# A spare PSUM bank for every second up step behind the attention, and x split in halves

## The reference

```python
scores = scale * np.matmul(q, k.transpose(0, 1, 3, 2))
kth = np.partition(scores, -top_k, axis=-1)[..., -top_k:-top_k + 1]      # top_k = 32
scores = np.where(scores >= kth, scores, -1000000000.0)
attn = softmax(scores)                                                   # over the last axis
x = (attn @ v), heads side by side                                       # 2304 tokens x 512
h = x @ w_in                                                             # 512 x 2048
g = np.where(h >= 1, h, np.where(h <= -1, 0.0, (h + 1) ** 2 / 4.0))
y = g @ w_out                                                            # 2048 x 512
h2 = np.maximum(y @ w_in2, 0.0)
out = h2 * h2 @ w_out2
```

## Time and profile before

| | |
|---|---|
| median of 3 runs | 1295.47 us (1295.22 to 1297.54) |
| the profiled execution | 1293.39 us |
| its span | 1291.6 us |
| PE busy | 1197.0 us, 93% |
| DVE busy | 910.0 us, 70% |
| POOL busy | 784.3 us, 61% |
| ACT busy | 720.0 us, 56% |
| DMA, mean | 189 GB/s over the span |

### The profile page before, as it was taken

The page is one execution under the profiler, slowest core; times in us unless marked ns, Lnnn a source line. Parts: engine busy times, 40 slices in busy tenths (PEclk is TensorE's granted clock), DMA queues, the critical chain, the costliest instruction groups (busy, mean ns, idle before and its releaser), DMA issues.

```text
span 1291.6 us, 24432 instructions
## 1 busy us (share of the span) xinstructions
PE 1197.0 (93%) x8760; PEld 1132.3 (88%) x8760; DVE 910.0 (70%) x2023; ACT 720.0 (56%) x1601; POOL 784.3 (61%) x637
## 2 busy tenths in 40 slices
PE   2677888999999999999999999999999999999998
PEld 1666878988888999999999999999989999998987
DVE  6789899988899998998889998988961111121111
ACT  4555556676555476767666655455543565643332
POOL 2999777786888767778666766666562222222222
PEclk9999899999999999999999999999999999999999
DMA  5899757575779962454427841456339400780000
GB/s 194 277 342 343 253 185 271 190 243 208 285 277 340 398 262 85 156 165 141 131 97 278 320 170 37 140 166 204 124 107 357 182 34 1 279 309 15 19 18 17
DMA packets 98728, 245.89 MB, mean 190 GB/s; under 512 B 7344, under 2 KB 48304, under 8 KB 86320
## 3 DMA queue, kind: packets, MB, share of 16 engines
q1 hardware_dynamic: 98608, 244.33, 53.6%
HBM read 167.23 MB, written 77.07 MB: 189 GB/s over the span
## 4 chain that ended last, share of the span: by engine, by line
PE 66%; POOL 13%; ACT 8%; DVE 6%; issue 4%; DMA 3%; SPq 0%; ACTq 0%; POOLq 0%
PE h_ps L569 26%; PE y_ps L590 13%; PE y_ps L584 11%; PE pv_ps L531 6%; POOL s_sb L1029 5%; POOL prob L1034 4%; PE tr_ps L504 3%; DVE top L847 2%; PE score_ps L469 2%; DVE rest L849 2%; POOL kq_lo L1013 2%; POOL w_out L1021 1%; ACT prob L687 1%; ACT s_sb L664 1%; POOL g_lo L1047 1%
## 5 line engine op out<-in xcount | busy, mean ns | idle before, releaser
L569 PE MATMUL h_ps<-xt_hi,w_in 128*128 128x256 f32 x2304 | 477.0, 290 | 8.0 <-DVE xt_lo L893 3.3
L1047 POOL TENSOR_TENSOR g_lo<-g_sb,g_hi 128x256 fp32r<-128x256 f32 x288 | 216.6, 752 | 411.2 <-ACT g_hi L765 411.1
L569 PEld LDWEIGHTS h_ps<-xt_hi,w_in 128*128 128x128 f32 x2304 | 379.4, 191 | 13.9 <-issue 4.8
L569 PE MATMUL h_ps<-xt_lo,w_in 128*128 128x256 f32 x1152 | 326.3, 283 | 0.0
L847 DVE MAX8 top<-rest 128x8 f32<-128x576 f32 x432 | 303.5, 743 | 0.0
L1029 POOL TENSOR_SCALAR s_sb<-s_sb,top 128x576 f32<-128x576 f32 x144 | 258.5, 1795 | 51.1 <-DVE top L847 50.1
L584 PE MATMUL y_ps<-g_hi,w_out 128*128 128x256 f32 x1152 | 231.7, 284 | 1.0 <-POOL g_lo L1047 0.8
L765 ACT ACTIVATE g_hi<-g_sb 128x256 fp32r<-128x256 f32 x288 | 120.8, 420 | 185.4 <-DVE g_sb L901 66.0
L569 PEld LDWEIGHTS h_ps<-xt_lo,w_in 128*128 128x128 f32 x1152 | 221.1, 192 | 2.3
L849 DVE MATCH_REPLACE8 rest<-top,rest 128x576 f32<-128x576 f32 x288 | 211.2, 739 | 0.0
L590 PE MATMUL y_ps<-w_out,g_hi 128*128 128x512 f32 x576 | 203.0, 394 | 0.1
(11 more groups left out here) (73 smaller groups left out, 1696.8 us busy)
## 6 DMA issues: line engine op xcount, KB each, us to landing
w_in<-w_scratch SPq DMA_DIRECT2D x32, 1024.0 KB, 6.9
w_out<-w_scratch SPq DMA_DIRECT2D x32, 1024.0 KB, 8.0
ks<-ks_scratch SPq DMA_DIRECT2D x47, 576.0 KB, 5.8
qs<-qs_scratch SPq DMA_DIRECT2D x78, 256.0 KB, 4.5
stage<-in_w_dram SPq DMA_DIRECT2D x32, 512.0 KB, 4.7
w_scratch<-w_in SPq DMA_DIRECT2D x16, 1024.0 KB, 6.9
w_scratch<-w_out SPq DMA_DIRECT2D x16, 1024.0 KB, 8.2
v_sb<-in_vv_dram SPq DMA_DIRECT2D x48, 325.0 KB, 5.6
```

The lines of the kernel that those rows point to most:

```text
L569: last = pe.matmul(h_ps[:, 0:CHUNK], wi[:, f // 2, w, m, cols], x[:, m, :], start=(m == 0 and n == 0), stop=(m == KT - 1 and n == 2))
L1047: pool.tensor_tensor(g_lo[k % 2][:, :], g_sb[k % 2][:, :], g_hi[k % 2][:, :].bitcast(F32), ALU.subtract).then_inc(g_lo_done, 1)
```

## The change

Up steps with an odd k whose position lies behind `ALONE` write to the first 256 columns of `score_ps` instead of `h_ps`, and their ReLU reads from there. Such a step waits for the last score copy and for ReLU k-2 instead of k-1; the even step behind it also waits for ReLU k-2 only. `split_x` becomes two ACT instructions and two DVE instructions of 512 columns each, `x_lo_done` counts two for each job, and the first up step of a job waits for the first half ahead of its matmuls m = 0 and for the second half ahead of m = 2.

```diff
+def own_bank(k):
+
+    return k % 2 == 1 and UP_POS[k] > ALONE
...
+        def h_bank(k):
+
+            return score_ps[:, 0:CHUNK] if own_bank(k) else h_ps[:, 0:CHUNK]
...
             def load_x(j):
-                sp.wait_ge(x_lo_done, j)
+                sp.wait_ge(x_lo_done, 2 * j)
...
             def up(k):
                 j, f = k // FT, k % FT
-                if k:
-                    pe.wait_ge(relu_done, k)
-                if f == 0:
-                    pe.wait_ge(x_lo_done, j + 1)
+                if own_bank(k):
+                    pe.wait_ge(s_copied, 2 * SLOTS)
+                    pe.wait_ge(relu_done, k - 1)
+                elif k:
+                    pe.wait_ge(relu_done, k - 1 if own_bank(k - 1) else k)
                 wait_block_ready(pe, k, "in")
                 cols = slice(P * (f % 2), P * (f % 2 + 1))
                 for m in range(KT):
+                    if f == 0 and m % 2 == 0:
+                        pe.wait_ge(x_lo_done, 2 * j + m // 2 + 1)
                     for n, (w, x) in enumerate(((0, xt_hi), (0, xt_lo), (1, xt_hi))):
-                        last = pe.matmul(h_ps[:, 0:CHUNK], wi[:, f // 2, w, m, cols], x[:, m, :],
+                        last = pe.matmul(h_bank(k), wi[:, f // 2, w, m, cols], x[:, m, :],
...
             def split_x(j):
                 act.wait_ge(x_loaded, 16 * (j - DIRECT + 1))
                 act.wait_ge(h_done, FT * j)
-                act.activation(xt_hi[:, :, :].rearrange("p m t -> p (m t)"), xr[:, :],
-                               ACT.Copy).then_inc(x_hi_done, 1)
+                for i in range(2):
+                    act.activation(xt_hi[:, 2 * i:2 * i + 2, :].rearrange("p m t -> p (m t)"),
+                                   xr[:, 2 * CHUNK * i:2 * CHUNK * (i + 1)], ACT.Copy).then_inc(x_hi_done, 1)
...
-                    act.activation(r[:, :], h_ps[:, 0:CHUNK], ACT.Relu).then_inc(relu_done, 1)
+                    act.activation(r[:, :], h_bank(k), ACT.Relu).then_inc(relu_done, 1)
...
             def split_x(j):
-                dve.wait_ge(x_hi_done, j - DIRECT + 1)
-                dve.tensor_tensor(xt_lo[:, :, :].rearrange("p m t -> p (m t)"), xr[:, :],
-                                  xt_hi[:, :, :].rearrange("p m t -> p (m t)").bitcast(F32),
-                                  ALU.subtract).then_inc(x_lo_done, 1)
+                for i in range(2):
+                    dve.wait_ge(x_hi_done, 2 * (j - DIRECT) + i + 1)
+                    m = slice(2 * i, 2 * i + 2)
+                    dve.tensor_tensor(xt_lo[:, m, :].rearrange("p m t -> p (m t)"),
+                                      xr[:, 2 * CHUNK * i:2 * CHUNK * (i + 1)],
+                                      xt_hi[:, m, :].rearrange("p m t -> p (m t)").bitcast(F32),
+                                      ALU.subtract).then_inc(x_lo_done, 1)
```

More of the change, by code:

```diff
@@ L750, in curve @@
                 if layer == 2:
-                    act.activation(r[:, :], h_ps[:, 0:CHUNK], ACT.Relu).then_inc(relu_done, 1)
+                    act.activation(r[:, :], h_bank(k), ACT.Relu).then_inc(relu_done, 1)
                     return
-                act.activation(r[:, :], h_ps[:, 0:CHUNK], ACT.Relu, bias=1.0).then_inc(relu_done, 1)
+                act.activation(r[:, :], h_bank(k), ACT.Relu, bias=1.0).then_inc(relu_done, 1)
                 if k >= 2:
@@ L960, in split_handed @@
                 dve.wait_ge(x_copied[1], c + 1)
-                dve.sem_inc(x_lo_done, 1)
+                dve.sem_inc(x_lo_done, 2)
             def slot(n):
```

## The result

The changed kernel takes 1287.16 us (median; 1285.3 to 1287.56) beside 1296.17 us for the one before: a ratio of 0.9934, 95% interval 0.9922 to 0.9947, by the ratio some 8.5 us less. The forecast was 4.0 us less, 1291.5, and its range began at 1289.0. The sign was right, the size was off by a factor of two.

The account below looks back on a forecast made before the run. TensorE (PE), busy 93% of the span, was taken as the bound; 1.47 + 2.13 + 0.1 + 0.3 = 4.0 us off the median 1295.47 gave 1291.5 us, range 1289.0 to 1294.5.

Parts of the forecast that it names:

- 0.71 us in layer 2: Job changes counted as layer 2 (jobs 15 to 17): second bank removes the whole 0.71 us each, 2.13 us in all.
- xt_lo's 0.05 in jobs 16 and 17: Layer 2 up steps 0.05 us too long behind a late xt_lo; halves give back 2 x 0.05 = 0.1 us.
- Extra satisfied waits: One added wait on the score copies in 53 odd up steps: taken as zero, upper bound 10.6 us.
- In layer 1 I had 0.49: Layer 1 job changes (jobs 12 to 14): net gain 0.49 us each after a new wait, 1.47 us in all.
- They don't move with PE: Layer 1, job 13: ACT's y_ps copies keep their time though PE comes 0.71 us earlier; first copy still ends at 1058.51.
- the new wait: Layer 1 job changes: down(k), opening a new sum in y_ps, waits 0.22 us for ACT's copy of the old one.
- whose chain runs through DVE and GpSimd and isn't moved: Slots: PE's waits for the masked prob, 0.81 and 1.14 us, stay and limit what the xt_lo halves gain.
- the term for PE's early start: Slots: PE starts some 0.5 us sooner on the first xt_lo half at three waits; 0.3 us taken.
- the bound of 1.5 us: Slots: most that PE's earlier starts could give, 3 x 0.5 us at its three waits for xt_lo.
- Rival (c): The slot stage passes all 1.5 us of PE's earlier starts on: 1290.3 us; chance 0.15.
- rival (a): Dearer DVE pieces land on the ranking in the slots, up to 1.6 us lost: 1293.4, no change; chance 0.13.
- the signs named ahead: Six L751/L753 waits gone; jobs 13, 14 about 46.3 us; three ys waits of 0.2; 32 xt_lo at 0.69, its wait shrinking.

Follow-up runs that it names:

- e8: The full change, but behind the slots ACT copies y_ps out one operation later, behind g_hi of the next step; 1288.95 us, ratio 0.9955 to the kernel before.
- e3: The full change (second bank and halves of x) measured once more against the kernel before; 1287.60 us, ratio 0.9947.
- e4: The full change, but PE waits for both xt_lo halves ahead of its first matmul; 1288.21 us, ratio 0.9949 to the kernel before.
- e9: The full change, with DVE's eight weight subtractions in two pieces too; 1298.12 us, ratio 1.0027 to the kernel before.
- e5: The full change, but xt_hi in one piece and only xt_lo in halves; 1286.56 us beside 1294.94 for the kernel before, ratio 0.9936.
- e12: The full change, with only GpSimd's long subtractions (weights, k and q) in two pieces too; 1291.60 us, ratio 0.9974 to the kernel before.

## Why the prediction was off

**The job changes: right in place, a term too small.** 0.71 us in layer 2 measured 0.72, three times. xt_lo's 0.05 in jobs 16 and 17 measured 0.05 and 0.07. Extra satisfied waits cost nothing: odd up steps stay at 1.43 and 1.44 us. In layer 1 I had 0.49 and it is 0.61 to 0.66. The failing step reads "They don't move with PE": I took the copy of y_ps at 1057.91 to be queued behind ACT's own work. ACT had been done with L759 sooner. This row of the kernel before stands right ahead of it:

```profile
1057.40 0.42 ACT L759 ACTIVATE g_sb<-g_sb 128x256 f32<-128x256 f32 x1
```

Its start lies 0.51 us ahead of the copy, while in the kernel after the two starts are 0.32 apart. The missing 0.19 was a wait for down(k-1), whose last matmul is recorded to 1057.88 and which now ends 0.71 sooner. So the copy moved by 0.19, and the new wait is 0.06 us instead of 0.22. That the copy is the next bound was right (e8). Six job changes gave 4.24 us in e3 (4.20 in the first trace), I had 3.70 with xt_lo's 0.1.

**The slots: one mechanism missing, the other too small.** I had 0.3 us, and 2.4 to 2.8 were there in columns 3 to 9; this is most of the miss. The step that failed is the one on the masked prob, "whose chain runs through DVE and GpSimd and isn't moved". It was moved: GpSimd's mask lay beside DVE's subtraction and waited for it. This kind of wait, at jobs 3 to 6, is 1.6 us (what e4 keeps), and my sum has no term for it. The rows to see it by were in the trace of before, had I looked at GpSimd there: 2.79 us where others take 1.72. I costed the pieces by DVE's and PE's time alone.

The second step is the term for PE's early start, 0.3 us, which measured 0.8 to 1.2. I had taken the bound of 1.5 us down because waits for the masked prob follow two of the three waits. At job 6 that was right: the wait of 0.24 us for xt_lo went, and the one for the prob grew from 1.14 to 1.33. The longest, 2.1 us at job 7, falls to 1.6, the 0.5 us that I had costed, and column 7 shows them and more in all traces with the early start but e9's. Rival (c), that the slots pass all 1.5 us on, so had the right mechanism for about two thirds of its size, and lacked the other one too. Its 1290.3 is still 3.1 us above what was measured. My rival (a), the dearer pieces on the ranking, has not come about: at job 3 a pair beside GpSimd costs DVE 0.5 us more and the operation behind gives that back.

**Small tiles.** The Trainium skill's page "VectorE: DVE Perf Modes" (The TRN2 errata) speaks against cutting an operation up, and for DVE's own time the rows agree (two pieces of 0.69 for one of 1.23). The time of the kernel went the other way, since what GpSimd and PE gained by the cut was more than what DVE paid for it.

**Of the signs named ahead,** the six waits are gone, xt_lo appears 32 times at a median of 0.69 us, and PE's wait for it shrinks from 3.3 to 2.0 us, as said. Jobs 13 and 14 lose 0.66 us and not 0.49, and no wait of 0.2 us for ys stands there, only the 0.06.

Open stays why the first measurement (8.5 us) is above the second (7.0 to 7.4), within the intervals, and what moves the first 380 us of a trace by a microsecond or more. The granted clock alone doesn't order them: e5 has TensorE at 1.2 GHz for 82 of the first 150 us and comes to its first split at 304.5 us, the kernel before has 10 us of it and 304.8, e12 has 3 and 307.5.

## What to carry to other kernels

Before costing a shortened or cut DVE operation, look at what GpSimd runs beside it: a GpSimd duration well above its usual one is a wait in disguise, and shortening the pieces that hold it off is a gain for whoever waits for GpSimd. Cut where what stands beside is urgent and holds DVE off only briefly, as the mask did (0.47 us of its 1.72). Leave whole where it is a long GpSimd operation with two inputs, since the second piece then waits for all of it (3.93 us for 1.70). The end of a cut can also decide who starts first: at job 4 0.1 us decided over 1.2 us on DVE. When a wait is removed, check of each "next" wait whether its starter is really its own queue, by comparing the distance of starts with an undisturbed pair.

## What the hardware showed that was not expected

A DVE operation on two SBUF tensors holds GpSimd's mask off for its whole length: the mask's loss was 1.07, 0.53 and 0.27 us for pieces of 1024, 512 and 256 columns. The other way round it depends on GpSimd's operation. Its subtractions and the masked prob, with two inputs, held DVE off to their end (2.84 us for a piece of 512 columns); the mask, with one input and a scalar, held it off for 0.47 us of 1.72, and DVE's further pieces then ran at full speed beside it. And a second PSUM bank is enough to take the whole 0.71 us of a job change in layer 2 away and 0.65 in layer 1, though only 0.46 of it stood in the trace as a gap: the restart costs half as much again.
